# Two early drains, 224 slots for an expert, constants in the setup, and gathers awaited tile by tile

## What is computed

```python
x = attention(q, k, v)                         # (3072, 512), local window 96 + 8 global keys
# first layer
do = x @ w_skip > 0                            # about half of the tokens
e_idx = argmax(x[do] @ w_gate);  gate = softmax(...)[e_idx]
for e in range(8):                             # any number of tokens for an expert
    h = maximum(xc[e_idx == e] @ w1[e], 0);  y = gate * (h @ w2[e])
x[do] += y
# second layer: every token, each expert exactly 3072 / 8 = 384
for idx in argsort(-(x @ w_gate).flatten()):   # greedy: best logit first, expert full at 384
    ...
for e in range(8):
    out[assigned == e] = maximum(x[assigned == e] @ w1[e], 0) @ w2[e]
```

## Time and profile before

| | us |
|---|---|
| median of 3 runs (lowest, highest) | 870.97 (869.21, 871.67) |
| the profiled execution | 873.73 |
| its span, first to last instruction | 871.9 |
| attention | 0 to 236.2 |
| first layer | 236.5 to 510.1 |
| second layer | 510.2 to 871.9 |
| busy in the span: PE, DVE, ACT, POOL | 758.9, 538.1, 457.4, 165.0 |

### The profile page before, as it was taken

How to read it: one execution, slowest core, us unless ns; L and a number is a source line. 1 busy time by engine, 2 the same in 40 slices (tenths; PEclk the granted TensorE clock), 3 DMA queues, 4 the chain that set the end, 5 groups by cost and what they waited for, 6 DMA issues and landing times. The chain is left out here.

```text
span 871.9 us, 15492 instructions
## 1 busy us (share of the span) xinstructions
PE 758.9 (87%) x5529; PEld 691.1 (79%) x5529; DVE 538.1 (62%) x1441; ACT 457.4 (52%) x919; POOL 165.0 (19%) x186
## 2 busy tenths in 40 slices
PE   0899999999739999999999911899999999999994
PEld 0799999998729998999999801879797888888893
DVE  3977678677467775665666327585756767675320
ACT  2789889888415443554554301535354555535350
POOL 5000000000020222022121121132324141423221
PEclk9999999999959999999999855899999999999998
DMA  8888999998273466345663003658676757769651
GB/s 180 177 196 210 258 211 275 214 266 249 101 244 126 149 218 234 109 150 200 228 212 113 5 10 118 183 175 213 203 190 235 187 189 182 211 176 302 193 110 39
DMA packets 66425, 157.93 MB, mean 181 GB/s; under 512 B 11542, under 2 KB 14998, under 8 KB 66336
## 3 DMA queue, kind: packets, MB, share of 16 engines
q1 hardware_dynamic: 54624, 121.05, 47.3%
q0 software_dynamic: 11712, 35.73, 16.9%
HBM read 119.11 MB, written 23.50 MB: 164 GB/s over the span
## 5 line engine op out<-in xcount | busy, mean ns | idle before, releaser
L1607 PE MATMUL r_ph<-r_xh,r_w1h 128*128 128x384 f32 x256 | 90.8, 355 | 0.0
L557 ACT ACTIVATE pr<-pr,nmx 128x232 f32<-128x232 f32 (+1 forms) x192 | 79.9, 467 | 17.0 <-DVE nmx L653 17.0
L1607 PE MATMUL r_ph<-r_xh,r_w1l 128*128 128x384 f32 x256 | 86.6, 338 | 0.0
L1607 PE MATMUL r_ph<-r_xl,r_w1h 128*128 128x384 f32 x256 | 86.3, 337 | 0.0
L992 PE MATMUL m_ph<-m_xh,m_w1h 128*128 128x256 f32 (+1 forms) x288 | 85.5, 297 | 0.8 <-DVE m_hl L1194 0.7
L1117 ACT ACTIVATE m_hh<-m_ph 128x256 fp32r<-128x256 f32 (+1 forms) x72 | 26.8, 372 | 111.9 <-PE m_ph L992 105.4
L992 PE MATMUL m_ph<-m_xl,m_w1h 128*128 128x256 f32 (+1 forms) x288 | 83.2, 289 | 0.0
L992 PE MATMUL m_ph<-m_xh,m_w1l 128*128 128x256 f32 (+1 forms) x288 | 83.1, 289 | 0.0
L430 PE MATMUL sc<-kk,qh 128*128 128x256 f32 x192 | 58.9, 328 | 23.7 <-DVE ql L631 23.7
L653 DVE CUSTOM_DVE_ANT_0 pr<-sc,bias 128x232 f32<-128x232 f32 (+1 forms) x192 | 64.9, 374 | 19.1 <-PE sc L431 18.6
L1621 PE MATMUL r_py<-r_w2h,r_hh 128*128 128x512 f32 x192 | 76.5, 398 | 0.0
(11 more groups left out here) (272 smaller groups left out, 1954.1 us busy)
## 6 DMA issues: line engine op xcount, KB each, us to landing
r_w<-moe_w SPq DMA_DIRECT2D x64, 512.0 KB, 5.2
m_w<-moe_w SPq DMA_DIRECT2D x36, 512.0 KB, 5.6
row_buf<-moe_w SPq DMA_DIRECT2D x9, 2048.0 KB, 8.7
r_w2l<-r_w POOLq DMA_DIRECT2D x32, 512.0 KB, 5.3
k_raw<-kI SPq DMA_DIRECT2D x32, 416.0 KB, 8.2
q_raw<-qT SPq DMA_DIRECT2D x32, 384.0 KB, 9.4
x_rows<-row_buf SPq DMA_DIRECT2D x8, 1536.0 KB, 8.9
vo<-vL SPq DMA_DIRECT2D x16, 384.0 KB
```

What stands on the lines that cost most here:

```text
L557: nc.scalar.activation(pr[n % PRS][:, t, lo:CW], pr[n % PRS][:, t, lo:CW], ACT.Exp, bias=nmx[n % PRS][:, t:t + 1], scale=-1.0).then_inc(ex ...
L1607: last = nc.tensor.matmul(ph[m % 4][:, 0:CAP], w[:, c, m * P:(m + 1) * P], x[:, c, :], start=(c == 0 and a == 0), stop=(c == KC - 1 and a ...
```

## The change

- Constants: the second layer's constants (`fullf`, `pen2`, `owner`, `left`, `shut`, `alive`, `steps_f`, `after`, `lane1`, `ids`) are made by GpSimd at the end of the attention's setup; `firstb` and `onesb` are those of the first layer. The waits for `filled` in the second layer are gone. The first `bests` reads the logits without the masking operation.
- 224 slots: a full block has tiles of 128 and 96 rows (ROWS1, WIDE1 = 224). Transposes, matmuls, copies, gathers and scatters of the second tile have 96 rows. Overflow starts at 225 tokens, with one more possible tile.
- Two drains: `g.drain()` on GpSimd before scatter(7) of the first layer, and in window 7 of the second layer after the last w2_low_part.
- Second layer, phase f in window k: `places` goes from slot 15 to 14; `slots` and `marks` come before h_low_part(7) instead of behind it; LAST_TURN goes from slot 24 to 28.
- `rows2` is written before `homes`; the scatter of an expert's first tile waits for a new semaphore `homed`. Each gathered tile has its own semaphore, and `turn` goes tile by tile: 4 transposes for each, the count for slice c at the last tile.

```diff
+ROWS1 = (128, 96)
+WIDE1 = sum(ROWS1)
-OVER = N // P - TT1
+OVER = N // P - 1
@@ attention setup, GpSimd
+                for dst, value in ((fullf, 0.0), (pen2, 0.0), (owner, 0.0), (left, float(CAP)), (shut, 0.0)):
+                    keep_link(g.memset(dst[:], value))
+                keep_link(g.tensor_copy(alive[:], first[:]))
+                for r in range(TRIES):
+                    keep_link(g.tensor_scalar(steps_f[:, r, :], lane[:, 0:CANDS], float(CANDS) ** -(r + 1), None, ALU.mult))
+                keep_link(g.tensor_tensor(after[:], lessb[:], ident[:], ALU.add))
+                keep_link(g.tensor_scalar(lane1[:], lane[:], 1.0, None, ALU.add))
...
@@ first layer
+            def rows_in(k, t):
+                return ROWS1[t] if isinstance(k, int) and k < E else P
...
                 z_scatter(E - 2, 0)
+                g.drain()
                 scatter(E - 1, 1)
...
-                            last = nc.tensor.transpose(pt[c % 2][:, t * P:(t + 1) * P], xg[s][:, t, c * P:(c + 1) * P], ident[:])
+                            r = rows_in(k, t)
+                            last = nc.tensor.transpose(pt[c % 2][:, t * P:t * P + r], xg[s][0:r, t, c * P:(c + 1) * P], ident[0:r, 0:r])
...
-                    one_block(k, k % 2, BLK, lambda chunks: turn(k + 1, (k + 1) % 2, chunks))
+                    one_block(k, k % 2, WIDE1, lambda chunks: turn(k + 1, (k + 1) % 2, chunks))
...
-                        v.tensor_copy(zo[s][:, 0:T, :], pt[0][:, BLK:BLK + T * E].rearrange("p (t e) -> p t e", e=E)).then_inc(z_kept, 1)
+                        for t in tiles(k):
+                            r = rows_in(k, t)
+                            last = v.tensor_copy(zo[s][0:r, t, :], pt[0][0:r, BLK + t * E:BLK + (t + 1) * E])
+                        last.then_inc(z_kept, 1)
@@ second layer
-            TOTAL, PLACES, TABLE, TURN = 12, H_SLOTS - 1, H_SLOTS + 7, H_SLOTS + 18
-            LAST_PLACES, LAST_TABLE, LAST_TURN = 5, 13, H_SLOTS + 8
+            TOTAL, PLACES, TABLE, TURN = 12, H_SLOTS - 2, H_SLOTS + 7, H_SLOTS + 18
+            LAST_PLACES, LAST_TABLE, LAST_TURN = 5, 13, H_SLOTS + 12
...
                 def scatter(k, t):
                     pool.wait_ge(y_kept, TT * k + t + 1)
+                    if t == 0:
+                        pool.wait_ge(homed, k + 1)
...
                     if k < E - 1:
                         gather(k + 1)
+                    else:
+                        g.drain()
...
                 def turn(k):
-                    pe.wait_ge(gathered, 16 * TT * (k + 1))
-                    for c in range(KC):
-                        if k:
-                            pe.wait_ge(h_high, FC * (k - 1) + 5 + c)
-                            pe.wait_ge(h_low, FC * (k - 1) + 5 + c)
-                        for t in range(TT):
+                    for t in range(TT):
+                        pe.wait_ge(gathered[t], 16 * (k + 1))
+                        for c in range(KC):
+                            if k and t == 0:
+                                pe.wait_ge(h_high, FC * (k - 1) + 5 + c)
+                                pe.wait_ge(h_low, FC * (k - 1) + 5 + c)
                             last = nc.tensor.transpose(ph[c][:, t * P:(t + 1) * P], xg[:, t, c * P:(c + 1) * P], ident[:])
-                        last.then_inc(x_turned, 1)
+                            if t == TT - 1:
+                                last.then_inc(x_turned, 1)
...
+                    v.tensor_tensor(rows2[:, f % E, :], parts[:, :, 1], tiles[:], ALU.add).then_inc(listed, 1)
                     link(v.scalar_tensor_tensor(out=homes[:, f % E, :], in0=parts[:, :, 1], scalar=astray[:, 0:1], in1=tiles[:], op0=ALU.add, op1=ALU.add))
-                    v.tensor_tensor(rows2[:, f % E, :], parts[:, :, 1], tiles[:], ALU.add).then_inc(listed, 1)
+                    dve.sem_inc(homed, 1)
...
-                dve.wait_ge(filled, FILLS)
-                bests()
+                bests(logits2)
...
                         h_low_part(k, 6)
-                        h_low_part(k, 7)
                         slots(f)
                         marks(f)
+                        h_low_part(k, 7)
                         listing(f)
```

More of the change, by code:

```diff
@@ L148, in build @@
         rows2 = sb("rows2", [P, E, CAP // P], I32)
+        fullf = sb("fullf", [P, CANDS], BF16)
+        pen2, owner = sb("pen2", [P, NT]), sb("owner", [P, NT])
+        left, shut, alive = (sb(x, [P, E]) for x in ("left", "shut", "alive"))
+        steps_f = sb("steps_f", [P, TRIES, CANDS])
+        after, lane1, onesb = sb("after", [P, P], BF16), sb("lane1", [P, P], BF16), onesb1
+        ids, idsf = sb("ids", [P, NT, 2], BF16), sb("idsf", [P, 2, NT])
         late = ExitStack()
@@ L811, in moved @@
                 return 16 * (TT1 * (k // 2 + 1) if isinstance(k, int) and k < E else k + 1)
+            def rows_in(k, t):
+                return ROWS1[t] if isinstance(k, int) and k < E else P
             def width(k):
-                return P * len(tiles(k))
+                return sum(rows_in(k, t) for t in tiles(k))
             def column_of(k, t):
@@ L1000, in y_products @@
                     for a, (h, w) in enumerate(((hh, w2h), (hh, w2l), (hl, w2h))):
-                        last = nc.tensor.matmul(py[t % 2][:], h[:, c, t * P:(t + 1) * P], w[:, c, :],
+                        r = rows_in(k, t)
+                        last = nc.tensor.matmul(py[t % 2][0:r, :], h[:, c, t * P:t * P + r], w[:, c, :],
                                                 start=(c == 0 and a == 0), stop=(c == FC - 1 and a == 2))
@@ L1060, in ahead @@
                         turn(E, 0, chunks)
-                one_block(E - 1, 1, BLK, ahead)
+                one_block(E - 1, 1, WIDE1, ahead)
                 with pe.If(n < 1):
@@ L1397, in build @@
             totals, incl, excl = (tb(x, [P, E, NT]) for x in ("tot", "incl", "excl"))
-            left, shut, need, cnt, alive, value = (tb(x, [P, E]) for x in ("left", "shut", "need", "cnt", "alive", "value"))
+            need, cnt, value = (tb(x, [P, E]) for x in ("need", "cnt", "value"))
             needc = tb("needc", [E, 1])
@@ L1424, in build @@
             polls, ranks_p = pb[:, 0:CANDS], pb[:, 128:128 + NT]
-            z_loaded, ended, turned, spread, filled = (sem(x) for x in ("z_loaded", "ended", "turned", "spread", "filled"))
+            z_loaded, ended, turned, spread = (sem(x) for x in ("z_loaded", "ended", "turned", "spread"))
             tried, met, judged, polled = (sem(x) for x in ("tried", "met", "judged", "polled"))
             chosen, summed, ruled, verdict = (sem(x) for x in ("chosen", "summed", "ruled", "verdict"))
-            owned, ranked, tabled, placed, listed = (sem(x) for x in ("owned", "ranked", "tabled", "placed", "listed"))
+            owned, ranked, tabled, placed, listed, homed = (sem(x) for x in ("owned", "ranked", "tabled", "placed", "listed", "homed"))
             posed, replied = sem("posed"), sem("replied")
@@ L1436, in build @@
             w2_low = [sem(f"w2_low{i}") for i in range(FC // 2)]
-            gathered, x_turned, x_high, x_low = (sem(x) for x in ("gathered", "x_turned", "x_high", "x_low"))
+            gathered = [sem(f"gathered{t}") for t in range(TT)]
+            x_turned, x_high, x_low = (sem(x) for x in ("x_turned", "x_high", "x_low"))
             h_done, h_high, h_low, y_done, y_kept, scattered = (
                 sem(x) for x in ("h_done", "h_high", "h_low", "y_done", "y_kept", "scattered"))
-            PHASES, FILLS = E - 1, 17
+            PHASES = E - 1
             POSED, ROUND_LINKS = 2 * ROUNDS + 2, 5
@@ L1474, in load2 @@
                             sp.wait_ge(w2_low[i], 16 * k)
[L1475 removed]
+                    for t in range(TT):
+                        sp.wait_ge(gathered[t], 16 * (k + 1))
                     for i in range(FC // 2):
```

120 lines of the change are left out of this document (51 added, 69 removed).

## The result

The changed kernel takes 848.85 us, median of four runs (845.71 to 851.72), for 870.68 us of the kernel before beside it. The ratio is 0.975, 95% interval 0.9707 to 0.9793. The forecast was 847.1 us. The four times lie in two pairs, 845.7 and 847.0 at a mean granted clock of 0.949 and 0.950, and 851.7 and 850.7 at 0.944 and 0.946.

The account below looks back on a forecast made before the run. TensorE was taken to bound the two expert layers, with waits for gathers and marks and idle joints. Gains of 6.1 + 2.8 + 1.6 + 5.9 + 7.5 = 23.9 us off 870.97 gave 847.1 us, range 841 to 859.

Parts of the forecast that it names:

- Constants: Start of second layer: VectorE's 2.47 us wait for GpSimd's constants and the masking operation L1780 go, 2.8 us gained.
- 224 slots: First layer's full blocks: 224 moving columns for 256 shorten the matmul spacing, 6.1 us gained, between 1 and 7.5.
- the floor: First layer's h products: something beside the columns keeps matmul spacing from falling under 111.5 ns, so 8.8 ns saved each.
- Drains: Ends of both layers: drains where GpSimd idles take on the cost of its earlier transfers, 7.5 us gained.
- First turn: Second layer's first expert: tiles turned as they land and gathers starting 0.26 us sooner, 1.6 us gained, between 0.9 and 2.
- the third rival: First layer: TensorE's granted clock falls in all seven z parts, costing 11.4 us, 858.5 us in all; chance 0.07.
- Windows: Second layer, windows k = 0 to 5: waits for third tile and marks shrink, 0.98 us each, 5.9 us together.
- The new wait at the rank product: Second layer's windows: the rank product moves ahead of its input, the scan upto, so TensorE waits about 0.2 us.
- shares: Ends of both layers: the cost is proportional to GpSimd's transfers, so the two drains gain 10.5 us.
- a line through the two layers: Ends of both layers: 0.9 us for 29 transfers, 31 ns each, so the drains gain 3.8 us.
- The first rival: Ends of both layers: a drain costs the same whatever lies before it, 854.6 us in all; chance 0.25.
- The other side: First layer: an expert with 225 to 256 tokens brings a second overflow block, some 35 us, 882 us; chance 0.03.

Follow-up runs that it names:

- run 4: The changed kernel with full blocks of 128 + 128 rows (256 slots) in place of 224: 853.7 us, ratio 0.9794.
- run 5: The changed kernel measured once more, unaltered, against the kernel before: 847.37 us, ratio 0.9733.
- run 6: The changed kernel with one semaphore for all three gathered tiles and the old turn, chunk by chunk: 852.84 us, ratio 0.9791.
- run 7: The changed kernel with count_extra's operations spread, and with rank product and marks back at their old places: 846.14 us, ratio 0.9712.
- Run 3: The kernel before with one drain only, in window 3 of the second layer behind its last w2_low_part: 868.27 us, ratio 0.9961.

## Why the prediction was right

The time and the sign held, and so did the mechanisms of the constants, the floor and the drains. The sizes of the drains, of the first turn and of the clock did not. Step by step:

- **224 slots**, 6.1 forecast. The floor was right to a tenth of a nanosecond, 111.4 for 111.5, and so was the size where the clock holds, 6.0 us (runs 4 and 5). The formula of the Trainium skill (TensorE: Matmul & The Clock Gate, section Back-to-back issue gap) would have had 9.7, an estimate; the trace does not bear it out at this width. The term that failed is the price of the hold in block 1. I had it at 0.3 us, as time that VectorE gives back. It is a lever on the clock: in some executions block 1 is 3.2 us longer (29.55 for 26.30), and the longer group of times, about 5 us above the shorter (851 for 846), has the lower clock. That is the third rival, at another place than I put it (not the z parts by themselves, whose blocks 4 to 7 kept their clock at 24.95 us) and in part only.
- **Constants**, 2.8 forecast, 2.75 measured, of which 2.4 is the wait and 0.4 the dropped operation.
- **First turn**, 1.6 forecast, 0.4 to 0.5 measured. Three things failed. I took off 1.5 from 2.82 us, the length of the twelve transposes, but the first product starts 2.48 us behind the first of them (549.83), so that 1.0 was to be had and not 1.3. The 0.26 for the row numbers did not arrive: the first gather starts 0.39 us sooner but takes 1.50 us for 1.16, and the third ends 5.46 us behind the copy of the tiles in both kernels. And I followed the tiles to x_high and forgot what VectorE does ahead of x_low: with the tiles turned sooner, the last step of the search (cmpf, until 539.4) ends later than x_high.
- **Windows**, 0.98 each forecast, 1.18 measured in the steady ones, and the seven together 5.8 to 6.9 us for 5.9. The split was right for the marks, 0.1 and 0.16. The new wait at the rank product did not appear in the result's profile. The turn undone alone costs 0.5 and not 0.88; what is left beside it fits the row numbers, which bring the third gather 0.8 us and not 0.26 forward (runs 6 and 7). I had averaged the waits of six windows; they are 0.7 in five and 1.6 in the sixth, where 0.9 stays.
- **Drains**, 7.5 forecast, 10.0 to 10.2 measured. The mechanism was right; the mis-sized step is the choice between shares (10.5) and a line through the two layers (3.8). The line came from lengths of 5.5 and 6.4 us, and these were the stretches that I had asked for the earlier trace rows, from 504.5 and 865.5 us on, not the joints. GpSimd's last transfers end at 503.93 and 863.02, and from there the lengths are 6.3 and 8.9 us: 2.6 us for 29 transfers, 90 ns each and not 31, which for 122 transfers would have given 11 us. So the lengths were not near each other, and my reason against shares was a misreading; the trace of the kernel before had the answer. Run 3, which changes the count inside one layer, gives 81 and 83 ns a transfer. The first rival, a drain that costs the same whatever lies before it, is refuted by the same run.
- **The other side**: the overflow block stayed one.

The sum of terms in an execution whose clock holds (run 5's profile) is 25.0 us of span. In the result's profile it is 21.9. The forecast of 23.9 lay between by errors that cancel: the drains too small by 2.5 us, the first turn too large by 1.2, and no term for the clock in block 1 (up to 3.2). That the number came so near is luck to this extent.

## What to carry to other kernels

Count the transfers that GpSimd issues in a Block, and place a drain where it idles, behind as many of them as can be; read the cost from the end of the last transfer on, and not from a stretch that looks empty. In a stretch bound by TensorE, look for chains on another engine that hold it for even 1 us, and spread them: where the clock falls behind the wait, that costs more than the wait. When a product with few columns takes far longer than its columns need, look at how far apart the columns lie in memory, and at what it costs the engine that writes them.

## What the runs showed of the hardware

- The end of a Block costs 81 to 83 ns for each transfer that GpSimd issued since its last drain, three times measured, for gathers and scatters of 96 or 128 rows and for transfers of 512 KB alike; a drain in a stretch where GpSimd idles takes this on at no cost that the span shows (10.2 us gained for 10.0 at the two ends).
- bf16 columns 48 bytes apart: 24 products of 120 columns took 5.06 us, 211 ns each; side by side 70 ns each, with the same strided weights.
- fp32r products of 224 and of 128 columns are spaced alike, 111.4 and 111.5 ns, at full clock.
- A hold of TensorE of 1.1 us had the clock fall from 2.4 to 1.2 GHz behind it in two of five profiled executions; one of 3.0 us in the one profiled, and by time and mean clock in all five; one of 0.7 us in none of four, and with the work spread in none of four.
